# Two early expert tiles, weight splits on GpSimd and reordered gate steps in a fused attention, mixture-of-experts and dense kernel

## The chip, the cores and the metric

The kernel runs on 1 core of one Trainium2 chip. The metric is the device time of one execution in microseconds. The kernel before was run three times: 1479.68, 1479.9 and 1480.39 us, so its median is 1479.9 us.

The engines are named by their jobs: TensorE (PE in the profile) multiplies matrices and transposes, and writes to PSUM; PEld is its weight load. VectorE is DVE, ScalarE is ACT, GpSimd is POOL; SyncE (SP) only issues transfers here. A small q behind an engine's name is its instruction sequencer.

## The reference

Three stages run one after the other, all in fp32.

```python
# attention between 512 tokens and 32 states, per batch (8) and head (8), width 64
a = softmax(scale * x @ state.T);  xread = a @ state
a2 = softmax(scale * state @ x.T); sread = a2 @ x
x = concat([xread, sread], axis=2)          # -> 4352 rows of 512: 8 batches of 544

# mixture of experts: 8 experts, 512 -> 1024 -> 512, one expert per row
logits = (x / |x|) @ (emb / |emb|).T / tau
e = argmax(logits);  gate = softmax(logits)[e]
x = gate * (relu(x @ w1[e]) @ w2[e])

# dense: 512 -> 2048 -> 512
r = relu(x @ w_in)
out = (s * r * r + b) @ w_out
```

With the inputs of the reference the experts get 851, 381, 299, 441, 934, 323, 655 and 468 rows, and in tiles of 128 rows 7, 3, 3, 4, 8, 3, 6 and 4, together 38. Of the 851 rows of expert 0, 714 lie in the first six batches.

## The kernel before

**Precision by splits.** TensorE multiplies in a narrower format, so each fp32 factor is split into a hi and a lo part. ScalarE makes `hi` by a copy that rounds (`x_hi`, `win_hi`, `split_hi`, `hidden_hi`), VectorE makes `lo = raw - hi` (`x_lo`, `win_lo`, `split_lo`, `hidden_lo`), and each product is hi by hi, hi by lo and lo by hi.

**Attention.** A loop over 8 batches is pipelined over the engines. In iteration i, TensorE does the scores of batch i (L1119), the ranks of batch i-2 (`ranks`, L1221), the state read of batch i-1, `state_emb(i)`, which waits for `pos_ready` of batch i-2, the transposes of the scores (L1144), the transposes of x of batch i+1 (L1102), and the token read of batch i-1 (L1190). ScalarE copies the x transposes out, does one exp over `e1`, 128x1024 (L587), then the copy of the state row (`row_t_evac`), the copies `a2_n` and the rows of batch i-1 (`rows_evac`, L559). VectorE does `place(i-2)`, `token_rows(i-1)`, the softmax steps, `state_logits(i-1)` and `choose(i-1)`. SyncE stores the rows of each batch to `x_tok` in HBM.

**Routing.** Each batch has a stage in which `choose` finds the expert of each row, `ranks` counts with two small matmuls how many rows of this expert came before, and `place` (L803 to L809) turns this into positions `pos5`. GpSimd then scatters the row numbers to `slot_tab` in HBM by five indirect DMAs (L478), one word per row. `pos5` is one buffer, so `place(bb)` waits until the slots of all batches before bb are written:

```python
if bb >= 1:
    dve.wait_ge(slots_written, 16 * (TPB + 1) * bb)
nc.vector.tensor_scalar(pos5[:], rank5[:], float(E * CAP), None, ALU.add).then_inc(pos_ready, 1)
```

After the last batch VectorE works out a table of tiles (`tile_tab`: the expert of each tile, whether it changes after it, its slot and its first row; L905 to L935). SyncE reads `slot_tab` back into `slot_sb` (L396), TensorE transposes it (L1265), VectorE copies it to `idx_all` (L939).

**Expert stage.** 38 tiles of 128 rows. `gather(g)` on GpSimd copies one column of indices and gathers 128 rows into `xg` (L492); it waits until the transposes (`xg_tr`), the sum of squares (`gate_sq`) and the logits (`gate_lg`) of the tile before have read `xg`. On TensorE `tile(g)` is `turn_hidden(g)`, `turn_x(g + 2)` (L1276), `up(g + 1)` (L1290), `down(g)` (L1316). On VectorE, it is `x_lo(g+2)`, `next_w1(g+1)`, `gate_final(g+2)`, `gate_logits(g+3)`, `hidden_lo(g+1)`, `gate_scale(g+3)`, `next_w2(g)`. `gate_scale` is a chain of 15 small steps on one column, each waiting for the one before (L993 to L999, the rsqrt steps at L748 to L753). `gate_soft(g)` on ScalarE waits for it. At a change of expert `next_w1` and `next_w2` split the next expert's weights, four hi and four lo parts of 128x1024 each (lo at L961 and L970), and `win_hi` and `win_lo` (L952) split one eighth of the dense weights `w_in`. SyncE loads the next expert's weights into one buffer, `w_raw`, as its halves come free.

The first expert's weights are split after attention: `split_hi` on ScalarE (L546, L550), `split_lo` on VectorE (L840, L844).

**Dense stage.** Tiles of up to 512 rows, `HEAD` = 2 blocks of 128 first. GpSimd adds up the 16 blocks of `w_out` for the bias (`b_row`, L512), VectorE makes `y_lo` (L1046) and `wo_lo` (L1041), TensorE does `dense_up` (L1357) and `dense_down` (L1376). GpSimd scatters the output rows to HBM (L524), and the program ends when the last of these has landed.

## Time and profile before

| | |
|---|---|
| median of three runs | 1479.9 us |
| the profiled execution, its own time | 1480.5 us |
| its span, first to last instruction | 1478.8 us |
| mean granted TensorE clock | 0.965 of full |
| TensorE matmul busy | 1365.8 us, 92% |
| VectorE busy | 651.3 us, 44% |
| ScalarE busy | 509.1 us, 34% |
| GpSimd busy | 149.0 us, 10% |

The rows below are taken from one profiled execution on the core. Times are in microseconds from the start of the span. In a row of the timeline the first two numbers are start and length of an instruction, or of several equal ones (x4), then come engine, line, operation and tiles, and in brackets how long the engine was idle before and what ended that. In the chain a row is a piece of the path that ended last. Busy shares of TensorE's matmuls include their pipelined ends.

### The profile page before, as it was taken

How to read it: one execution, taken by the hardware profiler on the slowest of the kernel's cores; microseconds unless marked ns; L12 is line 12 of the kernel's file. 1: busy time of each engine (PE TensorE's matmuls, PEld its weight loads, DVE VectorE, ACT ScalarE, POOL GpSimd, SP SyncE). 2: the span in 40 equal slices, each digit the busy share in tenths (PEclk: the TensorE clock that was granted, in tenths of full speed). 3: DMA queues.
4: the chain of work that ended last, by engine and by line, in shares of the span. 5: the costliest groups of instructions: out<-in, count | busy, mean ns of one | idle time of the engine just before them, and what ended most of it. 6: DMA issues, size and time to landing. Idle time of an engine off the chain costs nothing.

```text
span 1478.8 us, 22719 instructions
## 1 busy us (share of the span) xinstructions
PE 1365.8 (92%) x6878; PEld 1118.7 (76%) x6879; DVE 651.3 (44%) x1646; ACT 509.1 (34%) x977; POOL 149.0 (10%) x196
## 2 busy tenths in 40 slices
PE   5887459999999999997999999999999999999995
PEld 4655338877787877876888888888888888888884
DVE  4776653566664466465632422423223232322322
ACT  3544413455453355353422222222222222222221
POOL 1222310000000000004000100101001010100101
PEclk9988669999999999999999999999999999999998
DMA  9745333144433144214010010101001010010000
GB/s 218 147 112 79 65 106 120 51 150 172 172 115 101 44 161 146 80 52 153 24 44 0 24 34 0 57 0 57 0 0 57 0 57 0 21 36 0 29 1 28
DMA packets 75154, 100.19 MB, mean 68 GB/s; under 512 B 43977, under 2 KB 44521, under 8 KB 74097
## 3 DMA queue, kind: packets, MB, share of 16 engines
q1 hardware_dynamic: 62448, 69.72, 16.7%
q0 software_dynamic: 7200, 20.08, 4.1%
q10 hardware_dynamic: 5472, 9.96, 1.8%
q8 instruction: 19, 0.31, 0.1%
q14 instruction: 15, 0.11, 0.0%
HBM read 71.24 MB, written 28.66 MB: 68 GB/s over the span
## 4 chain that ended last, share of the span: by engine, by line
PE 74%; DVE 7%; DMA 5%; issue 5%; ACT 3%; DVEq 2%; ACTq 1%; POOL 1%; SPq 0%; another core or an unknown queue 0%; POOLq 0%
PE bank_a L1357 25%; PE bank_n L1376 13%; PE bank_t L1376 12%; PE bank_a L1290 9%; PE bank_n L1316 8%; DMA xg<-x_tok,g_idx 3%; PE bank_t L1301 1%; DMA slot_tab<-ids,pos 1%; DMA x_tok<-st_rows 1%; DVEq L339 1%; PE bank_a L1102 1%; PE bank_n L1276 1%; DVEq L336 1%; PE bank_t L1119 1%; DVE w_lo L970 1%
## 5 line engine op out<-in xcount | busy, mean ns | idle before, releaser
L1054 DVE TENSOR_TENSOR sq<-rel 128x512 f32<-128x512 f32 (+1 forms) x144 | 95.5, 663 | 484.8 <-ACT rel L714 484.8
L714 ACT ACTIVATE rel<-bank_a 128x512 f32<-128x512 f32 (+1 forms) x144 | 82.8, 575 | 549.6 <-PE bank_a L1357 549.6
L1357 PE MATMUL bank_a<-y_hi,w_in_hi 128*128 128x512 f32 (+1 forms) x576 | 218.6, 379 | 7.1 <-DVE y_lo L1046 7.0
L1357 PE MATMUL bank_a<-y_hi,w_in_lo 128*128 128x512 f32 (+1 forms) x576 | 217.9, 378 | 0.0
L1357 PE MATMUL bank_a<-y_lo,w_in_hi 128*128 128x512 f32 (+1 forms) x576 | 217.8, 378 | 0.0
L1357 PEld LDWEIGHTS bank_a<-y_hi,w_in_hi 128*128 128x128 f32 x576 | 109.0, 189 | 28.7 <-DVE y_lo L1046 7.5
L1357 PEld LDWEIGHTS bank_a<-y_lo,w_in_hi 128*128 128x128 f32 x576 | 109.0, 189 | 20.7 <-issue 0.2
L1357 PEld LDWEIGHTS bank_a<-y_hi,w_in_lo 128*128 128x128 f32 x576 | 108.9, 189 | 19.9
L1316 PE MATMUL bank_n<-w_hi,hid_hi 128*128 128x512 f32 x304 | 118.4, 389 | 1.9 <-DVE hid_lo L977 1.9
L1316 PE MATMUL bank_n<-w_hi,hid_lo 128*128 128x512 f32 x304 | 118.3, 389 | 0.0
L1376 PE MATMUL bank_n<-wo_hi,g_hi 128*128 128x512 f32 x288 | 112.6, 391 | 0.2 <-DVE g_lo L1057 0.2
L1376 PE MATMUL bank_n<-wo_lo,g_hi 128*128 128x512 f32 x288 | 112.2, 390 | 0.0
L1376 PE MATMUL bank_n<-wo_hi,g_lo 128*128 128x512 f32 x288 | 112.1, 389 | 0.0
L524 POOL DMA_INDIRECT out_rows<-w_raw,out_id x34 | 36.5, 1075 | 690.2 <-DVE w_raw L1066 685.0
L1290 PE MATMUL bank_a<-w_hi,xg_hi 128*128 128x512 f32 x304 | 100.1, 411 | 1.6 <-DVE xg_lo L948 1.4
L1376 PE MATMUL bank_t<-wo_hi,g_hi 128*128 128x512 f32 x256 | 100.8, 394 | 0.0
L1376 PE MATMUL bank_t<-wo_hi,g_lo 128*128 128x512 f32 x256 | 99.7, 389 | 0.0
L1376 PE MATMUL bank_t<-wo_lo,g_hi 128*128 128x512 f32 x256 | 99.6, 389 | 0.0
L1057 DVE TENSOR_TENSOR g_lo<-sq,g_hi 128x512 fp32r<-128x512 f32 (+1 forms) x144 | 95.5, 663 | 6.7
L1290 PE MATMUL bank_a<-w_hi,xg_lo 128*128 128x512 f32 x304 | 95.9, 397 | 0.0
L1316 PE MATMUL bank_n<-w_lo,hid_hi 128*128 128x512 f32 x304 | 81.7, 400 | 8.8 <-DVE w_lo L970 8.4
L718 ACT ACTIVATE g_hi<-rel 128x512 fp32r<-128x512 f32 (+1 forms) x144 | 87.7, 609 | 4.6
(202 smaller groups left out, 2065.7 us busy)
## 6 DMA issues: line engine op xcount, KB each, us to landing
w_raw<-in_moe_w SPq DMA_DIRECT2D x16, 2048.0 KB, 9.3
moe_tok<-yg ACTq DMA_DIRECT2D x38, 256.0 KB, 2.0
x_tok<-x_rows SPq DMA_DIRECT2D x8, 1088.0 KB
x_m<-in_x SPq DMA_DIRECT2D x8, 1024.0 KB
y_rows<-moe_tok SPq DMA_DIRECT2D x8, 1024.0 KB
win_raw<-in_moe_w_in SPq DMA_DIRECT2D x8, 512.0 KB, 8.9
w_raw<-in_moe_w_out SPq DMA_DIRECT2D x1, 4096.0 KB
slot_tab<-ids,pos POOLq DMA_INDIRECT x40
```

Of the source, the lines that this page charges most:

```text
L336: return eng.value_load(tile_tab[0:1, ds(g, 1)], min_val=0, max_val=E - 1)
L339: return eng.value_load(tile_tab[0:1, ds(NSLOT + g, 1)], min_val=0, max_val=1)
L524: nc.gpsimd.indirect_dma_start(out=out[:, :], out_offset=bass.IndirectOffsetOnAxis(ap=out_id[:, r:r + 1], axis=0), in_=o_sb[:, k, :], in_o ...
L714: nc.scalar.activation(rel[:, k, 0:cols], ps_g[k][:, 0:cols], ACT.Relu).then_inc(rel_ready, 1)
L718: nc.scalar.activation(g_hi[:, k, 0:cols], rel[:, k, 0:cols], ACT.Square).then_inc(g_hi_done, 1)
L970: nc.vector.tensor_tensor(w2_lo[:, c], w_raw[:, WCOLS + k * SLOT:WCOLS + (k + 1) * SLOT], w2_hi[:, c], ALU.subtract).then_inc(w2_ready, 1)
L1054: nc.vector.tensor_tensor(sq[:, 0:cols], rel[:, k, 0:cols], rel[:, k, 0:cols], ALU.mult).then_inc(sq_ready, 1)
L1057: nc.vector.tensor_tensor(g_lo[:, k, 0:cols], sq[:, 0:cols], g_hi[:, k, 0:cols], ALU.subtract).then_inc(g_ready, 1)
L1290: last = nc.tensor.matmul(ps_h[j][:], a[:, xc], w[:, c * F + j * BANK:c * F + (j + 1) * BANK], start=(c == 0 and a is xg_hi and w is w1_hi ...
L1316: last = nc.tensor.matmul(ps_y, a[:, kc], w[:, k * D:(k + 1) * D], start=(k == 0 and a is hid_hi and w is w2_hi), stop=(k == FC - 1 and w ...
L1357: last = nc.tensor.matmul(ps_g[n % 2][:, 0:cols], w[:, wc], a[:, c, 0:cols], start=(c == 0 and w is w_in_hi and a is y_hi), stop=(c == DC ...
L1376: last = nc.tensor.matmul(ps_o[TROWS - rows + r], a[:, n % 2, rc], w[:, wc], start=(n == 0 and a is g_hi and w is wh), stop=(n == FC2 - 1 ...
```

## The change

- `EARLY` = 2 tiles are filled from the rows of the first six batches (`SOON` = 6). After the slots of batches 0 to 5 are written, SyncE reads the first 256 slots of expert 0 into `idx_soon`; GpSimd gathers tiles 0 and 1 from them, between `write_slots(6)` and `write_slots(7)`. TensorE runs `up(0)`, `up(1)`, `down(0)` and `down(1)` around the last ranks, the slot transposes and the transposes of tile 2, which stand between the hi and the lo part of one of these each. Should expert 0 have fewer than 256 rows in those batches, `room` holds the lacking number: later rows are moved behind it, and the table and the copies of the ids take it into account.
- `split_hi(i)` moves into iteration i of attention on ScalarE. `split_lo` moves from VectorE to GpSimd, in front of `write_slots(k - 2)`.
- VectorE does `gate_logits(0)` and `x_lo(0)` ahead of `choose(B - 1)`, `gate_scale(0)` ahead of `place(B - 1)`. In a tile `gate_scale(g + 2)` stands directly behind `x_lo(g + 2)`, and `gate_final` at the end.
- `win_hi` and `win_lo` move from `next_w1` to `next_w2`, and SyncE loads w2 ahead of the piece of `w_in`.
- The first rows of the dense stage are loaded ahead of `w_out`.
- In the rsqrt step `y*y*n2` is formed as `y*n2*y`.

```diff
 # SyncE
+                if bb == SOON:
+                    sp.wait_ge(slots_written, 16 * (TPB + 1) * SOON)
+                        sp.dma_start(idx_soon[:], slot_tab[0:EARLY * P, :].rearrange("(t p) o -> p (t o)", p=P)).then_inc(soon_loaded, 16)
...
-            sp.wait_ge(gathered, 16)
+            sp.wait_ge(gathered, 16 * (EARLY + 1))
+            sp.wait_ge(st_stored, 16 * B)
             load_win(0)
             for e in range(1, E):
                 sp.wait_ge(w1_ready, WS * e)
                 sp.dma_start(w_raw[:, 0:WCOLS], w1[e].rearrange("(c p) n -> p c n", p=P)).then_inc(w1_loaded, 16)
+                sp.wait_ge(w2_ready, WS * e)
+                sp.dma_start(w_raw[:, WCOLS:2 * WCOLS], w2[e].rearrange("(c p) n -> p c n", p=P)).then_inc(w2_loaded, 16)
                 sp.wait_ge(win_ready, e)
                 load_win(e)
-                sp.wait_ge(w2_ready, WS * e)
-                sp.dma_start(w_raw[:, WCOLS:2 * WCOLS], w2[e].rearrange("(c p) n -> p c n", p=P)).then_inc(w2_loaded, 16)
 # GpSimd
-            for bb in range(B):
+            def split_lo(k):
+                if k < WS:
+                    pool.wait_ge(w1_hi_done, k + 1)
+                    c = slice(k * SLOT, (k + 1) * SLOT)
+                    nc.gpsimd.tensor_tensor(w1_lo[:, c], w_raw[:, c], w1_hi[:, c], ALU.subtract).then_inc(w1_ready, 1)
+                else:
...
+            def write_slots(bb):
                 pool.wait_ge(pos_ready, bb + 1)
                 for t in range(TPB + 1):
...
+            for k in range(2 * WS):
+                split_lo(k)
+                if k >= 2:
+                    write_slots(k - 2)
+            write_slots(B - 2)
+            pool.wait_ge(soon_loaded, 16)
+            pool.wait_ge(rows_stored, 16 * SOON)
+            pool.wait_ge(st_stored, 16 * SOON)
+            gather(0)
+            gather(1)
+            write_slots(B - 1)
             pool.wait_ge(rows_stored, 16 * B)
             pool.wait_ge(st_stored, 16 * B)
+            pool.wait_ge(tab_ready, 1)
             pool.wait_ge(idx_ready, 1)
-            gather(0)
-            pool.wait_ge(tab_ready, 1)
-            gather(1)
             gather(2)
 # ScalarE, attention loop
                 nc.scalar.activation(e1[:], e1[:], ACT.Exp, scale=-1.0).then_inc(e1_done, 1)
+                split_hi(i)
                 if i >= 1:
                     row_t_evac(i - 1)
...
-            for k in range(2 * WS):
-                split_hi(k)
 # ScalarE, first tiles
+            x_hi(0)
             gate_square(0)
-            x_hi(0)
             gate_soft(0)
-            act.wait_ge(tab_ready, 1)
             gate_square(1)
             hidden(0)
             x_hi(1)
-            next_w1(0)
+            hidden_hi(0)
+            hidden(1)
+            act.wait_ge(st_stored, 16 * B)
+            result(0)
+            act.wait_ge(tab_ready, 1)
+            store(0)
+            hidden_hi(1)
+            next_w1(1)
+            x_hi(2)
 # VectorE, rsqrt step, place, end of attention
-                    link(nc.vector.scalar_tensor_tensor(t, y, y, n2, ALU.mult, ALU.mult))
+                    link(nc.vector.scalar_tensor_tensor(t, y, n2, y, ALU.mult, ALU.mult))
...
+                if bb == SOON:
+                    route_step(nc.vector.tensor_scalar(room[:, 1:2], bank_l[:, L_SUM:L_SUM + 1], float(EARLY * P), None, ALU.min))
...
+                if bb >= SOON:
+                    route_step(nc.vector.scalar_tensor_tensor(rank5[:], hot5[:, :, 0], room[:, 0:1], rank5[:], ALU.mult, ALU.add))
...
             place(B - 2)
             token_rows(B - 1)
             state_logits(B - 1)
+            dve.sem_inc(hid_t_ready, HB)
+            gate_logits(0)
+            x_lo(0)
             choose(B - 1)
+            gate_scale(0)
             place(B - 1)
+            gate_logits(1)
+            x_lo(1)
+            hidden_lo(0)
+            gate_final(0)
...
             nc.vector.tensor_copy(tile_tab[:], tab_o[:]).then_inc(tab_ready, 1)
-            for k in range(WS):
-                split_lo(k)
             dve.wait_ge(slot_tr, 1)
             nc.vector.tensor_copy(idx_all[:], bank_r[:, E:E + 3 * TQ]).then_inc(idx_ready, 1)
-            for k in range(WS, 2 * WS):
-                split_lo(k)
+            gate_scale(1)
+            hidden_lo(1)
 # VectorE, a tile
             def tile(g):
                 x_lo(g + 2)
+                gate_scale(g + 2)
                 next_w1(g + 1)
-                gate_final(g + 2)
                 gate_logits(g + 3)
                 hidden_lo(g + 1)
-                gate_scale(g + 3)
                 next_w2(g)
+                gate_final(g + 2)
 # TensorE
             turn_x(0)
-            up(0)
+            up(0, last_ranks)
+            turn_hidden(0)
             turn_x(1)
+            up(1)
+            down(0, turn_slots)
+            turn_hidden(1)
+            down(1, lambda: turn_x(2))
             pe.wait_ge(tab_ready, 1)
+            up(2)
+            turn_x(3)
             last_g = last_tile(pe)
-            tile(0)
-            with pe.Fori(1, last_g) as g:
+            with pe.Fori(2, last_g) as g:
                 tile(g)
```

The second argument of `up` and `down` is called between their hi and their lo part. Tile 0 uses other PSUM banks (`ps_xt0`, `ps_y0`). Five table steps are added behind `o_row`, and the `moe_id` copies become ten instead of eight.

## Rows read from the trace of the kernel before

**Rows 1.** The page's 40 slices of the span, TensorE: busy tenths
```profile
PE   5887459999999999997999999999999999999995
```

**Rows 2.** Windows: us, busy us (count) of each engine, PEclk, DMA
```profile
176.00:202.00 26.00, 2.10 (x8) 1.41 (x9) 16.12 (x32) 2.63 (x5) 8.27 (x9) 0.50 0.17 48
```

**Rows 3.** The chain that ended last, 157 to 203 us: start, length, what
```profile
160.93 0.18 DVE pos L809
...
166.48 8.64 DMA slot_tab<-ids,pos
...
175.22 0.18 DVE pos L809
...
180.95 8.79 DMA slot_tab<-ids,pos
...
195.01 4.19 DMA xg<-x_tok,g_idx
...
201.76 1.65 PE bank_a L1290 x3
```

**Rows 4.** Timeline of ScalarE: the exp of e1 in batches 2, 5, 6, 7
```profile
55.40 1.06 ACT L587 ACTIVATE e<-e 128x1024 f32<-128x1024 f32 x1
...
111.86 1.05 ACT L587 ACTIVATE e<-e 128x1024 f32<-128x1024 f32 x1
...
130.93 1.06 ACT L587 ACTIVATE e<-e 128x1024 f32<-128x1024 f32 x1 [0.63 <-issue]
...
150.60 1.06 ACT L587 ACTIVATE e<-e 128x1024 f32<-128x1024 f32 x1 [4.70 <-DVE e L869]
```

**Rows 5.** Timeline of GpSimd and VectorE: slot scatters and pos
```profile
57.20 0.87 POOL L478 DMA_INDIRECT slot_tab<-ids,pos  x1 [0.30 <-issue]
...
68.04 0.17 DVE L809 TENSOR_SCALAR pos<-rank 128x5 int32<-128x5 f32 x1 [0.30 <-DMA slot_tab<-ids,pos]
...
125.64 0.17 DVE L809 TENSOR_SCALAR pos<-rank 128x5 int32<-128x5 f32 x1
...
151.07 0.86 POOL L478 DMA_INDIRECT slot_tab<-ids,pos  x1 [0.30 <-issue]
```

**Rows 6.** GpSimd's adds for b_row: ns min/median/max, first and last start
```profile
L512 POOL TENSOR_TENSOR b_row<-b_row,w_raw x14: 1262/1274/1607, 686.0 to 703.6; 128x512 f32<-128x512 f32 x14
```

**Rows 7.** Timeline of GpSimd: the last scatter of output rows
```profile
1468.17 0.97 POOL L524 DMA_INDIRECT out_rows<-w_raw,out_id  x1 [0.30 <-issue]
```

**Rows 8.** Timeline of TensorE: lo part of up(0), transposes of gathered tiles
```profile
208.37 1.98 PE L1290 MATMUL bank_a<-w_lo,xg_hi 128*128 128x512 f32 x8
...
228.80 0.60 PE L1276 MATMUL bank_n<-ident,xg 128*128 128x128 f32 x4
...
241.01 0.60 PE L1276 MATMUL bank_n<-ident,xg 128*128 128x128 f32 x4
...
302.18 0.60 PE L1276 MATMUL bank_n<-ident,xg 128*128 128x128 f32 x4
...
316.92 0.60 PE L1276 MATMUL bank_n<-ident,xg 128*128 128x128 f32 x4
```

**Rows 9.** Timeline of VectorE: gate_scale and w2 splits at a change
```profile
306.00 0.15 DVE L993 TENSOR_REDUCE gc<-lg 128x1 f32<-128x8 f32 x1
...
309.13 0.17 DVE L999 RECIPROCAL gc<-gc 128x1 f32<-128x1 f32 x1
...
310.75 4.63 DVE L970 TENSOR_TENSOR w_lo<-w_raw,w_hi 128x1024 fp32r<-128x1024 f32 x4 [1.46 <-ACT w_hi L631]
```

**Rows 10.** Timeline of VectorE and TensorE ahead of the dense stage
```profile
694.17 1.33 DVE L751 SCALAR_TENSOR_TENSOR gc<-gc 128x1 f32<-128x1 f32 x1
...
701.91 0.69 DVE L1046 TENSOR_TENSOR y_lo<-bank_r,y_hi 128x512 fp32r<-128x512 f32 x1 [1.79 <-issue]
...
690.50 0.49 PE L1316 MATMUL bank_n<-w_hi,hid_hi 128*128 128x512 f32 x1 [1.90 <-DVE hid_lo L977]
...
703.25 0.58 PE L1357 MATMUL bank_a<-y_hi,w_in_hi 128*128 128x256 f32 x1 [7.03 <-DVE y_lo L1046]
```

More of the change, by code:

```diff
@@ L379, in _ @@
                 sp.dma_start(x_tok[bb * ROWS + S:bb * ROWS + ROWS, :], st_rows[:]).then_inc(st_stored, 16)
+                if bb == SOON:
+                    sp.wait_ge(slots_written, 16 * (TPB + 1) * SOON)
+                    with nc.allow_non_contiguous_dma(reason="one word per row"):
+                        sp.dma_start(idx_soon[:], slot_tab[0:EARLY * P, :].rearrange("(t p) o -> p (t o)", p=P)).then_inc(soon_loaded, 16)
             w_in_s = w_in.rearrange("(c p) n -> p c n", p=P)
@@ L503, in _ @@
             gather(3)
-            with pool.Fori(1, last) as g:
+            gather(4)
+            with pool.Fori(2, last) as g:
                 gather(g + 3)
@@ L668, in _ @@
             x_hi(1)
-            next_w1(0)
+            hidden_hi(0)
[7 more added lines that the diff above has]
+            x_hi(2)
             gate_soft(1)
             gate_square(2)
-            hidden_hi(0)
+            result(1)
+            store(1)
+            gate_soft(2)
+            gate_square(3)
+            hidden(2)
+            x_hi(3)
+            next_w1(2)
+            gate_soft(3)
+            hidden_hi(2)
+            gate_square(4)
             win_hi(0)
+            next_w2(1)
             last = last_tile(act)
@@ L685, in tile @@
                 next_w2(g)
-            tile(0)
-            with act.Fori(1, last) as g:
+            with act.Fori(2, last) as g:
                 tile(g)
@@ L1013, in _ @@
             gate_scale(1)
-            x_lo(1)
-            next_w1(0)
+            hidden_lo(1)
+            next_w1(1)
+            gate_logits(2)
+            x_lo(2)
             gate_final(1)
-            gate_logits(2)
             gate_scale(2)
-            hidden_lo(0)
+            gate_logits(3)
+            gate_final(2)
+            x_lo(3)
+            gate_scale(3)
+            next_w1(2)
+            hidden_lo(2)
+            gate_logits(4)
             win_lo(0)
+            next_w2(1)
@@ L1021, in _ @@
+            gate_final(3)
             last = last_tile(dve)
@@ L1024, in tile @@
                 x_lo(g + 2)
+                gate_scale(g + 2)
                 next_w1(g + 1)
-                gate_final(g + 2)
                 gate_logits(g + 3)
                 hidden_lo(g + 1)
-                gate_scale(g + 3)
                 next_w2(g)
-            tile(0)
-            with dve.Fori(1, last) as g:
+                gate_final(g + 2)
+            with dve.Fori(2, last) as g:
                 tile(g)
@@ L1259, in _, with last_ranks, turn_slots @@
             row_logits(B - 1)
-            ranks(B - 1)
-            nc.tensor.matmul(bank_r[:, 0:E], ones_b[:], pre5[:, TPB + 1, :], start=True, stop=True).then_inc(tot_mm, 1)
-            pe.wait_ge(slot_loaded, 16)
-            pe.wait_ge(tab_link, 1)
-            for k in range(3):
-                last = nc.tensor.transpose(bank_r[:, E + k * TQ:E + (k + 1) * TQ], slot_sb[:, k, :], ident[0:TQ, 0:TQ])
-            last.then_inc(slot_tr, 1)
+            def last_ranks():
+                ranks(B - 1)
+                nc.tensor.matmul(bank_r[:, 0:E], ones_b[:], pre5[:, TPB + 1, :], start=True, stop=True).then_inc(tot_mm, 1)
+            def turn_slots():
+                pe.wait_ge(slot_loaded, 16)
+                pe.wait_ge(tab_link, 1)
+                for k in range(3):
+                    last = nc.tensor.transpose(bank_r[:, E + k * TQ:E + (k + 1) * TQ], slot_sb[:, k, :], ident[0:TQ, 0:TQ])
+                last.then_inc(slot_tr, 1)
             def turn_x(g):
@@ L1302, in turn_hidden, with down @@
                     last.then_inc(hid_tr, 1)
-            def down(g):
-                e = 0 if starts(g) else expert_of(pe, g)
-                if not starts(g):
+            def down(g, between=None):
+                e = 0 if isinstance(g, int) and g < EARLY else expert_of(pe, g)
+                if starts(g):
+                    pe.wait_ge(pos_ready, B)
+                elif not (isinstance(g, int) and g < EARLY):
                     pe.wait_ge(yg_ready, g)
+                dst = ps_y0 if starts(g) else ps_y
                 for w, done, factors in ((w2_hi, w2_hi_done, (hid_hi, hid_lo)), (w2_lo, w2_ready, (hid_hi,))):
+                    if between and w is w2_lo:
+                        between()
                     for k in range(FC):
```

204 lines of the change are left out of this document (116 added, 88 removed).

## The prediction

> **What bounds the kernel now.** I read the page of the profile first: TensorE is busy nine tenths or more from slice 7 to the end, with a hole in slices 4 and 5 and a dent in slice 18 [rows 1]. The windows size the hole: from 176 to 202 us TensorE works 2.1 of 26 us, at half clock [rows 2]. The chain says what fills it: position numbers, slot scatter, its landing, read-back, index, gather, first expert tile [rows 3]. Outside that, the expert stage has a steady period of 228.80 to 241.01 = 12.21 us, longer at the seven changes of expert [rows 8], and before the dense stage TensorE waits 7.03 us [rows 10]. The attention stage is not bound by TensorE: it is a loop over several engines, in which the exp of `e1` on ScalarE comes once a batch (call its start X, counted X2 for i = 2) [rows 4].
>
> **Splits in attention.** Eight hi halves move into attention behind that exp. They have the exp's shape, 128x1024, so 1.06 us each [rows 4]. The eight lo halves move from VectorE, where they lay under the slot wait (so removing them gives nothing), to GpSimd. Nearest row: 128x512 on GpSimd takes 1.27 us [rows 6], so 2.55 us each; bounds 1.3 (no growth with size) and 3.2 (twice its slowest, 1.607).
>
> What matters is who queues behind them. In GpSimd's order `write_slots(k-2)` now stands behind `split_lo(k)`, which waits for `split_hi(k)`, which runs after exp of batch k. Before, the fifth scatter of a batch was issued 5.55 us after `pos` (160.93 to 166.48 [rows 3]), thus about at X. Now `pos` has long been there, and GpSimd gets to it at X + 1.06 (exp) + 1.0 (split hi) + 2.55 = X + 4.6; the fifth goes out some 5.5 later, at X + 10.1. It then has to land, and `place(bb)` still waits for all slots of the batches before bb ahead of writing `pos5`. Landing, from the start of the fifth issue: 8.64 and 8.79 us in the chain [rows 3]; 10.8 in batch 0 (from 57.20 to the wait of `pos` that ended at 68.0, under other transfers); at most 9.9 for batch 5 (151.07, and `pos` at 160.93 did not wait) [rows 3, 5]. Another scatter, of the output, also has 10.6 us from its issue to the end of the span [rows 7]. I take L = 9.2, bounds 8.64 and 10.8.
>
> In batch i+1, `place(i-1)` thus ends at X(i) + 10.1 + L, where before it ended 13.8 us after X (111.86 to 125.64). TensorE's `state_emb` waits for `pos`, and the score transposes and x transposes behind it lead to the next exp: 125.64 to 130.93 = 5.2 us [rows 4, 5]. So the period becomes 15.3 + L = 24.5 us, against 19.1 and 19.7 before (111.86, 130.93, 150.60 [rows 4]). From X2 = 55.40 + 1 = 56.4: four periods to X6 = 154.2, one shorter by 1.05 (the last has no x transposes) to X7 = 177.6, before 150.60. After the loop, `place(6)` waits for slots of batch 5: 177.6 + 10.1 + 9.2 = 196.9, where before it was 160.93. This is **+36** (L = 8.64: +32.6; 10.8: +45.6). Without this wait the hi splits alone would have given some +7.
>
> By the Trainium skill, page "DMA: Bandwidth & Descriptors", section "Anatomy of one DMA", a GpSimd DMA costs about 2 us plus its bytes; the period would stay below 20 us and this term would be 7. The trace's 8.64 and 8.79 disagree with it, and I go by them.
>
> **Early tiles.** Expert 0 has 714 rows in six batches (counted from the reference's inputs), over 256, so `room` is 0 and there are still 38 tiles. What they gain is TensorE work under the last slot wait. From `pos` of batch 6 (p): five scatter issues 6.5, index copy and its hand-over 1.3, then from the gather's issue to the first matmul 6.75 (195.01 to 201.76 [rows 3], of it 4.19 the landing) give the start T of `up(0)` at p + 14.6; p + 20 if the gather queues behind the slot scatter. VectorE now waits for that gather before `choose(7)`, which waited for no gather before: all the last routing comes behind it. `last_ranks` comes behind the hi part of `up(0)`, 6.6 us at half clock (201.76 to 208.37 [rows 3, 8]), so the last `pos` is at T + 8.0. From there to the next gathered tile (now tile 2) it took 24.0 (175.22 to 195.01 + 4.19 [rows 3]): T + 32.0. Under it TensorE does `up(0)`, `up(1)`, `down(0)`. Then a second wait: VectorE copies the indices at T + 26.4 and only then does `gate_scale(1)`, 3.3 us (306.00 to 309.13 + 0.17 [rows 9]), and `hidden_lo(1)`; `down(1)` starts at T + 31, runs 5.5 (under half a period of 12.21) plus the transposes between its halves, `up(2)` starts at T + 37. It runs 5.5, and gathers 3 and 4, each released only by the transposes before it, put the transposes ahead of `up(3)` at T + 47.6 = p + 62.2. Before, that point was 241.01 - 160.93 = 80.1 after p [rows 3, 8]. Gain **-17.9**. The five extra table steps and two more `moe_id` copies lie under these waits; uncovered they would cost 1.2 and a few us.
>
> So the stage ends 36 - 18 = **+18** later (bounds +14.7 and, with L = 10.8 and the queued gather, +33).
>
> **Changes of expert.** Before, the transposes at 302.18 and 316.92 lie 14.74 apart, 2.5 over the period; TensorE waits for `w_lo` of w2, whose four splits start at 310.75 behind `gate_scale` (3.3 us) [rows 8, 9]. With `gate_scale(g+2)` moved ahead of them they start about 1.9 earlier (gather and `gate_soft` come 1.4 later, which eats the rest of 3.3). `win_lo` now stands behind them and before the next `x_lo`: 1.2 us (a quarter of the 4.63 of the four splits), which takes back 0.8. Seven times 1.1 = **-8** (bounds 0 and -17.7, the whole excess). In a plain tile ScalarE's chain is longer by the waited `gate_soft`; `hidden_hi` comes 2 us later and still 0.9 before `down` needs it, so nothing. If that cover is short, 31 tiles pay it.
>
> **Dense start.** TensorE waits until 703.25 because the last `gate_scale` is stretched: its steps with two inputs take 1.3 us (694.17) rather than 0.2 while GpSimd adds up `b_row`, and `y_lo` comes at 701.91 [rows 10]. The same steps now come before `hidden_lo(37)`, just as the adds start: the stretch delays `down(37)` instead, from 690.5 [rows 10] to some 697, and the dense stage starts 1 to 2 us earlier. **-1.5** (bounds -7.03, stretch gone; +2). The earlier row loads were done in time before: nothing.
>
> The Trainium skill, page "GPSIMD Engine Reference", section "Key points", says that GpSimd contends with VectorE instructions of two SBUF inputs. The trace agrees (1.30 us against 0.22); by that rule the new operand order of the rsqrt step, still two inputs, changes nothing here.
>
> **Sum.** 1480.5 (the profiled run, span 1478.8 plus 1.7) + 18 - 8 - 1.5 = 1489.0; the median of the runs is 0.6 below the profiled one, so 1488.
>
> **Rivals.**
> 1. *The gather queues behind the slot scatter and landings are 10.8*: 1480.5 + 33 - 8 - 1.5 = 1504. For: 10.8 was seen under load. Against: scatters are issued 1.27 us apart and yet land together.
> 2. *Faster: the scatters land in time.* If L is 5 or less, `place` no longer waits in the loop (period 15.3 + L against the 20 of the loop with splits). Then attention gives +7, the last slot landing is 5 us shorter, and the stage ends 16 earlier: 1480.5 - 16 - 8 - 1.5 = 1455. What the Trainium skill's page says of about 2 us would be this case. Against: four rows between 8.64 and 10.8. It turns into a gain from L = 6 or so downwards.
> 3. *Faster: forecast path, but the changes and the dense start give all they can*: +14.7 - 17.7 - 7 = 1470.5.
> 4. *No change*: +14.7, 2.0 saved per change, 1.6 at the dense start: 1480.
>
> **Numbers.** Forecast 0.50, rival 1 0.15, rival 2 0.10, rival 3 0.12, rival 4 0.08; 0.05 for a stall that I don't see, slower. About 0.2%, 3 us, is what a measurement can tell: slower 0.70, same 0.08, faster 0.22. The range 1470 to 1509 leaves out rival 2 and some 0.05 above; the forecast alone spans 1483 to 1499.
>
> **What would show it.** Right: exps of `e1` some 24 us apart from batch 2 on; VectorE's `pos` waiting for `slot_tab` in batches 3 to 7; the last exp near 178; `up(0)` near 211 with a wait for slots inside `down(0)`; transposes at a change 13.6 apart. Wrong: periods of 20 us (the landing is hidden, rival 2); `pos` waiting over 11 us; a plain tile above 12.3 us, from the later `hidden_hi`; the stretched steps gone from VectorE.

## The result and the profile after

The kernel after takes 1558.7 us (median of 4, 1557.0 to 1561.0), the kernel before 1479.8 on the same chip: ratio 1.0534, 95% interval 1.0516 to 1.0553. It is slower, as forecast, but by 79 us where 8 were forecast, and outside the range. The profiled span is 1556.8 us against 1478.8, 78.0 more.

TensorE's row of the page's 40 slices (tenths busy in slices of 38.9 us) shows where:

```profile
PE   3754663799999999999799999999999999999995
```

Slices 0 to 6 are now thin, not only 4 and 5 [rows 1]; from slice 8 on the page looks as before. The windows give batches 2 to 6 in one row (length, busy us and count of PE, PEld, DVE, ACT and POOL, granted clock, DMA share, GB/s):

```profile
74.00:220.00 146.00, 82.10 (x664) 61.51 (x664) 73.80 (x175) 50.27 (x112) 36.09 (x30) 0.74 0.48 65
```

TensorE is busy 56% of the time, and no engine more. Where no engine is near full, the engines wait for one another in a circle. Two timelines and the chain close it: the exp of `e1` on ScalarE (compare [rows 4]), `pos` on VectorE, and one batch of the chain.

```profile
37.70 1.05 ACT L635 ACTIVATE e<-e 128x1024 f32<-128x1024 f32 x1
...
73.50 1.05 ACT L635 ACTIVATE e<-e 128x1024 f32<-128x1024 f32 x1
104.34 1.05 ACT L635 ACTIVATE e<-e 128x1024 f32<-128x1024 f32 x1
136.13 1.06 ACT L635 ACTIVATE e<-e 128x1024 f32<-128x1024 f32 x1
163.59 1.05 ACT L635 ACTIVATE e<-e 128x1024 f32<-128x1024 f32 x1
...
219.46 1.06 ACT L635 ACTIVATE e<-e 128x1024 f32<-128x1024 f32 x1 [13.68 <-DVE e L927]
```

```profile
97.48 0.17 DVE L877 TENSOR_SCALAR pos<-rank 128x5 int32<-128x5 f32 x1 [11.81 <-DMA slot_tab<-ids,pos]
129.72 0.17 DVE L877 TENSOR_SCALAR pos<-rank 128x5 int32<-128x5 f32 x1 [13.00 <-DMA slot_tab<-ids,pos]
157.19 0.17 DVE L877 TENSOR_SCALAR pos<-rank 128x5 int32<-128x5 f32 x1 [7.41 <-DMA slot_tab<-ids,pos]
...
242.15 0.17 DVE L877 TENSOR_SCALAR pos<-rank 128x5 int32<-128x5 f32 x1 [10.41 <-DMA slot_tab<-ids,pos]
267.57 0.17 DVE L877 TENSOR_SCALAR pos<-rank 128x5 int32<-128x5 f32 x1
```

The chain that ended last (start, length, what) runs once round the circle:

```profile
136.13 0.47 ACT e L635
...
137.08 1.07 ACT w_hi L598
...
138.22 2.34 POOL w_lo L505
...
140.72 1.00 POOL slot_tab L512
...
145.94 11.16 DMA slot_tab<-ids,pos
...
157.19 0.18 DVE pos L877
...
157.51 0.60 PE bank_l L1201 x8
158.11 1.90 PE bank_n L1213 x8
160.01 2.52 PE bank_a L1171 x12
...
163.59 0.48 ACT e L635
```

Read it as exp, hi split, lo split, five scatters, landing, `pos`, score and x transposes, exp. The periods are 30.8, 31.8, 27.5, 28.3 and 27.6 us.

Three points of the span split the 78.0 us. `pos` of batch 6 comes at 242.15 instead of 160.93 [rows 3]: **+81.2**. The transposes ahead of up(3) come 69.3 us after it (row below) instead of 80.1 [rows 3, 8]: **-10.7**. From there to the last gathered tile it is 439.7 us instead of 434.3, **+5.4**, and from there to the first product of `dense_down` 34.9 instead of 32.6, **+2.3**. The rest is equal.

```profile
296.64 0.60 PE L1352 MATMUL bank_n<-ident,xg 128*128 128x128 f32 x4
306.41 0.66 PE L1352 MATMUL bank_n<-ident,xg 128*128 128x128 f32 x4 [1.02 <-DMA xg<-x_tok,g_idx]
311.49 0.66 PE L1352 MATMUL bank_n<-ident,xg 128*128 128x128 f32 x4 [2.69 <-DMA xg<-x_tok,g_idx]
```

### The profile page after: what moved, and what is told of

The parts are those of the page before. It is cut to its first block, busy times and chain, and to the rows that moved or that the text cites. A ratio compares the mean times of both kernels' runs of the same rounds, so it can differ in the third digit from the quotient of the medians.

```text
span 1556.8 us, 22584 instructions
## 1 busy us (share of the span) xinstructions
PE 1385.7 (89%) x6879; PEld 1133.9 (73%) x6880; DVE 660.3 (42%) x1633; ACT 508.1 (33%) x977; POOL 169.7 (11%) x208
## 4 chain that ended last, share of the span: by engine, by line
PE 64%; DMA 9%; issue 7%; DVE 6%; ACT 5%; POOL 3%; ACTq 3%; SPq 1%; DVEq 1%; POOLq 0%
PE bank_a L1448 24%; PE bank_n L1467 13%; PE bank_t L1467 11%; PE bank_n L1401 6%; PE bank_a L1370 5%; DMA slot_tab<-ids,pos 5%; DMA xg<-x_tok,g_idx 4%; POOL slot_tab L512 2%; PE bank_a L1171 1%; DVE gc L813 1%; ACTq L345 1%; PE bank_t L1381 1%; PE bank_n L1213 1%; DVE gc L815 1%; ACTq L348 1%
## 5 line engine op out<-in xcount | busy, mean ns | idle before, releaser
L1401 PEld LDWEIGHTS bank_n<-w_hi,hid_hi 128*128 128x128 f32 x296 | 57.2, 193 | 36.4 <-issue 22.1
## 6 DMA issues: line engine op xcount, KB each, us to landing
x_tok<-x_rows SPq DMA_DIRECT2D x8, 1088.0 KB, 10.1
```

Of the source, the lines that this page charges most:

```text
L1401: last = nc.tensor.matmul(dst, a[:, kc], w[:, k * D:(k + 1) * D], start=(k == 0 and a is hid_hi and w is w2_hi), stop=(k == FC - 1 and w i ...
```

## The experiments

Of a1 to a4, b1 and e3 there is one execution each, and only terms of several us are read from it: three of the kernels below have the same attention code and reach `pos` of batch 6 at 164.8, 167.5 and 172.0 us. Chips differ too: the kernel before took 1479.8 us on the chip of the result, 1476.5 on that of a1 to a4, so a difference of 2 or 3 us in their spans is not read. Times are told beside that of the kernel before on the same chip; the kernel after is 78.9 above it.

**A late start (a1).** VectorE's first reduction stands in the timeline with this wait, which the prediction had not seen:

```profile
32.43 1.28 DVE L914 TENSOR_REDUCE nb<-s_t 128x1 f32<-128x512 f32 x2 [12.92 <-POOL late L495]
```

VectorE waits for three new memsets on GpSimd, and these stand behind GpSimd's wait for the cleared slot table. The edit puts the memsets first:

```
-            pool.wait_ge(tab_cleared, 16)
             nc.gpsimd.memset(first_e[:], 0.0).then_inc(tab_zero, 1)
             ...
+            pool.wait_ge(tab_cleared, 16)
```

> The changed kernel, with the four small memsets for first_e and late ahead of GpSimd's wait for the cleared slot table instead of behind it. Theory (a wait that the forecast missed: VectorE's first attention step waits for these memsets, and they wait for the transfer that clears slot_tab): the first exp of e1 returns from 37.70 to about 26, and the whole is 11 to 12 us shorter, 1546. Rival (the start is late because of the loads, and the memsets lie under them): the first exp stays near 37 and the time near 1558.

Measured: 1543.4 us beside 1476.5, so 66.9 above the kernel before instead of 78.9; the span is 15.1 shorter than after. The first exp is at 25.01 (37.70 after, 25.85 before), and the theory holds. The late start costs more than itself: the next two periods are 14.56 and 16.30 us here (14.56 and 14.99 before) and were 17.63 and 18.17 after, with a granted clock of 0.94 from 25 to 56 us here and 0.78 from 37 to 74 after. X2 is at 55.87, 17.6 sooner than after (e3 below, also without the late start, has it at 56.24).

**Who stands first on GpSimd (a2).**

```
             for k in range(2 * WS):
-                split_lo(k)
                 if k >= 2:
                     write_slots(k - 2)
+                split_lo(k)
```

> The changed kernel, with write_slots(k-2) ahead of split_lo(k) in GpSimd's order. Theory (the slot scatter standing behind the split is what stretches attention): pos waits for no slots any more in batches 3 to 7, the exps of e1 come 18 to 21 us apart instead of 27 to 32, pos of batch 6 comes near 187 instead of 242.15, and the time is 50 to 58 us shorter, about 1503. Rival (the splits themselves, the hi half on ScalarE and the contention of GpSimd with VectorE, stretch it): the periods stay above 25 us and the time above 1540.

Measured: 1499.0 us beside 1476.5, 22.5 above it instead of 78.9, so 56 us less (59.5 in the span) from swapping two lines. `pos` of batch 6 is at 182.04, the periods are 19 to 21 us. In its timeline of VectorE `pos` waits for no slot any more:

```profile
103.67 0.17 DVE L877 TENSOR_SCALAR pos<-rank 128x5 int32<-128x5 f32 x1
123.64 0.17 DVE L877 TENSOR_SCALAR pos<-rank 128x5 int32<-128x5 f32 x1
144.63 0.17 DVE L877 TENSOR_SCALAR pos<-rank 128x5 int32<-128x5 f32 x1
```

**The same order on the kernel before (e3).** It gets the splits in attention and nothing else of the change: the `split_hi(i)` behind the exp, and on GpSimd

```
+            for k in range(2 * WS):
+                split_lo(k)
+                if k >= 2:
+                    write_slots(k - 2)
```

> The kernel before with one part of the change alone: the splits of expert 0 in the attention loop, the low half on GpSimd ahead of the slots of batch k-2. There is no late start here and there are no early tiles. My theory, that this order alone makes the cycle exp, split, slots, landing, positions, exp: periods of 27 to 31 us, the positions of batch 6 some 55 us later than 160.9, and the time 1525 to 1535 us. The rival, that the early tiles' traffic or the added waits lengthen the landings: periods as forecast (24.5 us) and 1510 to 1516 us.

Measured: 1542.8 us beside 1477.1. `pos` of batch 6 is at 225.91, 65.0 us later than [rows 3]; the periods are 28 to 32 us. Two landings in its chain:

```profile
157.50 12.94 DMA slot_tab<-ids,pos
...
187.00 12.74 DMA slot_tab<-ids,pos
```

So the order alone makes the circle and its long landings. My number for `pos` was 10 us too small and the time lies 8 us above my range; the mechanism and place are right, and the rival (traffic of the early tiles) is out: there are none here, and the landings are 10.9 to 15.6 us, 13.2 on average.

**Why the landing is long (a4).** After, the scatters of a batch (140.72 to 145.94) go out together with SyncE's store of 1088 KB of token rows (issued at 141.96, median 10.1 us to landing; 5.9 in a2). The edit holds that store, and with it what SyncE has queued behind it (the state row and the next load of x), until the slots of the batches before are written:

```
+                if bb >= 1:
+                    sp.wait_ge(slots_written, 16 * (TPB + 1) * bb)
                 sp.dma_start(x_dst(bb), x_rows[:]).then_inc(rows_stored, 16)
```

> The changed kernel, with SyncE's store of the rows of a batch waiting until the slots issued before it have landed, so that scatter and store are no longer in flight together. Theory (the scatters land in 11 to 15 us instead of 8.6 to 8.8 because they now meet the row store): from the fifth issue to the end of pos's wait falls to about 9 us. Rival (they land late for a reason of their own): it stays at 12 or more. The time itself gets longer under both, by 5 to 50 us, since the store is now on the path of each batch.

Measured: 1548.7 us beside 1476.5, 72.2 above it instead of 78.9, span 9.8 *shorter*, against my forecast of longer. From the fifth issue to the end of the wait of `pos`:

| batch | 1 | 2 | 3 | 4 | 5 | 6 | mean |
|---|---|---|---|---|---|---|---|
| after | 14.1 | 15.6 | 11.3 | 12.4 | 12.4 | 12.9 | 13.1 |
| a4 | 8.8 | 7.3 | 6.0 | 12.9 | 10.5 | 8.0 | 8.9 |

```profile
118.79 0.17 DVE L879 TENSOR_SCALAR pos<-rank 128x5 int32<-128x5 f32 x1 [2.85 <-DMA slot_tab<-ids,pos]
143.90 0.17 DVE L879 TENSOR_SCALAR pos<-rank 128x5 int32<-128x5 f32 x1 [2.16 <-DMA slot_tab<-ids,pos]
175.78 0.17 DVE L879 TENSOR_SCALAR pos<-rank 128x5 int32<-128x5 f32 x1 [8.43 <-DMA slot_tab<-ids,pos]
```

(The table's a4 for batch 6 is 222.56 to 230.57.) With SyncE's transfers out of the way the landings are some 4 us shorter on average. The counts of DMA packets in windows show what the transfers do, and what they don't. In a4 the last packet of a scatter has moved 2 to 3 us after the fifth issue; after, with the store under way, 128 of the 160 packets of batch 4 move together between 176 and 177 us, up to 3.6 us after the issue at 173.38, and in the other batches the last ones move 4 to 8 us after it. Behind that comes a stretch of 4 to 11 us in which no packet of the scatter moves, in both kernels, before the wait of `pos` ends. It is what makes batch 4 of a4 long (windows 163 to 165 and 165 to 175.7 us; the wait ends at 175.78):

```profile
q0 software_dynamic: 64, 0.00, 2.0%
...
DMA packets 1, 0.01 MB, mean 1 GB/s; under 512 B 0, under 2 KB 0, under 8 KB 0
```

(The one packet is an instruction fetch. In the kernel before there is no packet at all from 184 to 189.7 us, the end of the landing of 8.79 [rows 3].) So SyncE's transfers explain some 4 of the 13.1 us. The longer part passes with none of the scatter's packets left to move, and why it takes 4 us once and 11 another time is open.

Of the 4.2 us gained per landing about 1.9 per batch reach `pos` of batch 6 (11.6 us sooner in all), for the path goes over the held queue now: the store of the state row stands behind the held one, and the next exp comes 8.3 to 9.3 us after `pos` instead of 5.4 to 6.9. From a4's chain:

```profile
137.86 5.94 DMA slot_tab<-ids,pos
...
144.23 4.80 DMA x_tok<-st_rows
```

**The order of the gate (a3).** VectorE's `gate_scale` goes back a tile ahead, `win_*` stays in `next_w2`:

```
             def tile(g):
                 x_lo(g + 2)
-                gate_scale(g + 2)
                 next_w1(g + 1)
+                gate_final(g + 2)
                 gate_logits(g + 3)
                 hidden_lo(g + 1)
+                gate_scale(g + 3)
                 next_w2(g)
-                gate_final(g + 2)
```

> The changed kernel, with VectorE's order in a tile as before (gate_final, gate_logits, hidden_lo, then gate_scale of the next tile but one), win_hi and win_lo still in next_w2. Theory (the new place of gate_scale loads the tiles around a change of expert and the last tile): excess over 12.25 us a tile falls from 23 to 18 or less, TensorE's 9.53 us wait in down of the last tile goes, total 5 to 8 us shorter, 1551. Rival (win_lo and the load order cause it): no more than 2 us.

Measured: 1556.1 us beside 1476.5, 79.6 above it; against my 5 to 8 us there is no gain that the times can tell. In the trace the excess over 12.25 us a tile falls from 23.2 to 22.2 us only, not to 18. At a change of expert, three intervals between transposes are 12.98, 12.88 and 13.64 us after, and 14.57, 12.86 and 12.25 in a3. Both are about 3 above the plain 36.75, where before it was 2.7. With `gate_scale` back, TensorE waits for `w_lo` as in the kernel before; with it ahead of the splits, ScalarE waits for the last step of `gate_scale`, with `gate_square`, `result` and `hidden_hi` queued behind, and TensorE then waits for `hid_lo` (0.74 us at 395.72). From the kernel after:

```profile
374.53 0.30 ACT L695 ACTIVATE pr<-sh,gc 128x8 f32<-128x8 f32 x1 [3.97 <-DVE gc L1001]
...
391.39 0.30 ACT L695 ACTIVATE pr<-sh,gc 128x8 f32<-128x8 f32 x1 [5.15 <-DVE gc L1001]
```

What a3 does mend is the dense start. After, the stretched gate steps stand ahead of `hidden_lo(37)` (VectorE, then TensorE):

```profile
763.74 1.30 DVE L813 SCALAR_TENSOR_TENSOR gc<-gc 128x1 f32<-128x1 f32 x1
765.26 1.12 DVE L815 TENSOR_TENSOR gc<-gc 128x1 f32<-128x1 f32 x1
```

```profile
773.99 0.79 PE L1401 MATMUL bank_n<-w_hi,hid_hi 128*128 128x512 f32 x1 [9.53 <-DVE hid_lo L979]
```

In a3 this wait is 1.90 us as before, and from the last gathered tile to the end it takes 803.3 us, before 803.5, after 805.6.

**The dense rows alone (c3).** The kernel before with `load_y(0, HEAD)` and `load_ids(0, HEAD)` ahead of the load of `w_out`.

> The kernel before, with only the loads of the first dense rows and their ids ahead of the load of the last weights. The prediction gave this part 1.5 us and no more than 7. Now I expect nothing: within 1 us of the kernel before, since TensorE waited 7.03 us at the first dense product for VectorE's y_lo, and after the change still 9.5 us for VectorE's hid_lo at the same place. The rival: 1.5 us or more faster.

Measured: ratio 1.0001 (0.9989 to 1.0013). Nothing, as the prediction's last sentence on the dense start had it.

**The terms together (b1, b2).** b1 is a1 and a2 in one kernel, b2 adds a3.

> The two largest terms taken away together: the small memsets ahead of the wait for the cleared table, and GpSimd writing the slots of batch k-2 before it splits piece k. If they are separate terms of the sum, they add: 1499.0 - 11.9 to 15 = about 1485 to 1487 us. The rival, that the late start was partly hidden behind the slot waits or behind the time of x: over 1492 us.

> The same with VectorE's gate_scale back a tile ahead, as before the change, in the loop over tiles. Two costs are then out of b1: ScalarE's waits for VectorE's reciprocal at a change of expert (some 0.2 us per change and one for up(3)), and gate_scale in the way of hid_lo at the start of the dense part (2.4 us). Expected 3 us below b1, about 1482 us, so level with the kernel before (1476.5 to 1480 us). The rival, that gate_scale costs only while the routing is late: the same as b1.

Measured: b1 1487.2 us beside 1482.5, 4.7 above it. a1 and a2 alone took off 12.0 and 56.4 of the 78.9, which would leave 10.5: together they are worth at least their sum. b2 1481.0 beside 1482.5, ratio 0.9992 (0.9976 to 1.0007). With three orders put right the whole change is worth nothing that can be measured.

**Where the lo split runs (b3).** From GpSimd back to VectorE, into its idle time between `r2` and the exp of `e1`:

```
                 nc.vector.reciprocal(r2[:], s2[:]).then_inc(sum2_steps, 1)
+                if i >= 1:
+                    split_lo(i - 1)
```

> b2 with the low halves split on VectorE, in its idle time before ScalarE's exp, instead of on GpSimd. My theory for what is left of the longer attention stage (some 1.3 us per batch): GpSimd's 2.34 us split stretches VectorE's small sum step from 0.18 to 2.1 us, and what follows waits for it. Then this step is back at 0.18 us, the batches are some 1 us shorter each, and the time is 6 to 9 us below b2. The rival, that ScalarE's 1.05 us high half ahead of its row copies is what lengthens a batch: no more than 2 us below b2, or above it, since VectorE has 1.23 us more in each batch.

Measured: ratio 0.9994 (0.9979 to 1.0008), the same as b2. The stretch is real and costs nothing that shows; in b2 and in b3 the small step is

```profile
97.07 2.12 DVE L936 TENSOR_SCALAR s<-s 128x32 f32<-128x32 f32 x1
```

```profile
97.76 0.18 DVE L936 TENSOR_SCALAR s<-s 128x32 f32<-128x32 f32 x1
```

and yet both have `pos` of batches 2 and 3 18.8 us apart (89.29 and 108.10; 90.03 and 108.83). My theory fell: the stretched step stood in the timeline, but the batch waits for something else, and for what was not followed up.

**The moved splits alone, slots first (e2).** e3 with the two lines swapped.

> The same part with the slots ahead of the split. It prices the moved splits alone, and so what the early tiles are worth in the kernel with three parts put right, which is level with the kernel before: there the path from the positions of batch 6 to up(3)'s transposes was 69.0 us against 80.1. If the early tiles give those 11 us by themselves, and the splits in attention cost 4 us and give nothing behind it, this kernel is 2 to 5 us slower than the kernel before. The rival, that part of the 11 us comes from the splits being out of the way behind the routing: level with the kernel before or faster.

Measured: ratio 1.0003 (0.9980 to 1.0027). `pos` of batch 6 is at 162.92, and up(3) 76.9 us behind it. So of the 11 us that b2 gains against 80.1 on that path, 3.2 come with the splits out of the way (2.5 in e3), 7.9 with the early tiles. b2 then loses 4.7 us of it again in the expert stage (439.4 us against 434.7), 2.1 of them in its first tile, 14.3 us long. That tile is long after too. The windows show a granted clock of 0.87 ahead of it, with TensorE busy 75%, 0.89 in it, and full speed (2.4 GHz) only from the next tile on; before, the same tile ran at 1.00. Below 1 the clock was for a part of the stretch at its lower level, 1.2 GHz:

```profile
258.00:311.00 53.00, 39.87 (x166) 30.58 (x166) 27.01 (x121) 12.48 (x30) 9.45 (x13) 0.87 0.38 135
```

```profile
311.00:326.00 15.00, 14.18 (x61) 11.61 (x62) 7.59 (x31) 4.94 (x13) 1.79 (x3) 0.89 0.18 54
326.00:338.00 12.00, 12.00 (x60) 10.03 (x59) 5.20 (x22) 4.21 (x11) 1.15 (x2) 1.00 0.17 52
```

**The gathers and the last routing (b4, c1, c2, e1, f1, g1).** After, the chain behind `pos` of batch 6 begins with this row, more than twice the 4.19 of [rows 3]:

```profile
249.03 9.28 DMA xg<-x_tok,g_idx
```

All six kernels start from b2. b4 puts `choose(7)` ahead of `gate_logits(0)` on VectorE and the last ranks ahead of tile 0 on TensorE.

> b2 with the choice of the last batch put ahead of the work of tile 0 on VectorE, and its ranks ahead of tile 0 on TensorE. My theory for the part of the early tiles' gain that did not come: VectorE and TensorE wait for gather(0), 9.3 us after its issue, with the last routing queued behind it. Then the last positions come some 8 to 11 us sooner, the last slots are issued right behind gather(1), about 5 us sooner, and so is up(3): 4 to 6 us below b2. The rival, that the two early tiles themselves fill that time: the same as b2.

Measured: 1478.9 us beside 1482.5, ratio 0.9968 (0.9948 to 0.9988), 2 us below b2 and not the 4 to 6 expected. The choice is done at 184.5, but the last `pos` comes only at 194.87, since `place(7)` still stood behind the gate of tile 0. Half the step was moved. c1 moves `place(7)` too, and the last slots ahead of the second gather:

```
             gather(0)
-            gather(1)
             write_slots(B - 1)
+            gather(1)
```

> The kernel with the choice first, but the last batch's routing is now finished ahead of tile 0 on every engine: VectorE places it before the logits of tile 0, and GpSimd writes its slots before it issues gather(1). There the choice was done at 184.5 us, and the positions still came at 194.87, behind the gate of tile 0. I expect the last positions some 8 us sooner, the slots in place some 7 us sooner, gather(1) some 1.5 us later and landing behind the slots; up(3)'s transposes 5 to 8 us sooner than 67 us after the positions of batch 6, so about 60, and the time 1471 to 1474 us where the kernel before has 1480. The rival, that gather(1), now behind the slots in its queue, holds up tile 1 by as much: no gain.

Measured: 1485.9 us beside 1482.8, ratio 1.0020 (1.0003 to 1.0037): slower, just clear of the noise, where 1471 to 1474 was expected; the rival had it. The last `pos` is 14.0 us behind that of batch 6 instead of 22.9, and it is all given back, because now gather(1) too is behind five scatters:

```profile
175.96 8.94 DMA xg<-x_tok,g_idx
...
190.58 9.48 DMA xg<-x_tok,g_idx
```

c2 puts gather(0) ahead of the slots of batch 6 and leaves gather(1) behind those of batch 7.

> c1 with gather(0) ahead of the slots of batch 6 on GpSimd, so that it has the queue for itself. If its 9.3 us to landing come from the five slot writes ahead of it, it lands some 4 us after its issue, about 10 us sooner, and tile 0 starts right behind the last ranks: 3 to 4 us below c1. If the landing stays near 9 us, it is the traffic of the row store, and c2 is 1 us below c1 or equal to it.

Measured: ratio 1.0025 (1.0009 to 1.0042), no better than c1 where 3 to 4 us were expected. gather(0) no longer holds anybody up; gather(1), issued at 190.80, takes 9.83 us and does. It is not the row store that holds it: no packet of SyncE's queue moves from 187 to 199 us. e1 puts both ahead: gather(0), slots of 6, gather(1), slots of 7.

> Gathers and slots in an order that keeps each gather clear of slots just issued: gather(0), slots of batch 6, gather(1), slots of batch 7, with the last batch placed ahead of tile 0 on VectorE and TensorE. In the kernels that were level or slower, a gather issued behind five slot writes landed 9.3 to 9.8 us later, one on a quiet queue 3.4 to 4.7 us later. So I expect gather(1) to land within 5 us, tile 1 to start some 10 us sooner than in c1, the last slots to be in place by 32 us after the positions of batch 6, and up(3)'s transposes about 60 us after them: 1470 to 1474 us, faster than the kernel before by 0.4% or more. The rival, that something behind the slots holds up tile 2 (the index table, the store's wait): up(3) at 66 to 70 us and level with the kernel before.

Measured: 1472.6 us beside 1477.1, ratio 0.9979 (0.9957 to 1.0001): half of the 0.4% expected, and not clear of no change. gather(1), issued at 178.27 with the slots behind it, has landed at 181.75, 3.5 us later. But `pos` of the last batch waits for the slots of batch 6, which went out behind a gather, with `x_lo(0)` queued behind it (VectorE's timeline):

```profile
177.05 0.17 DVE L877 TENSOR_SCALAR pos<-rank 128x5 int32<-128x5 f32 x1 [4.60 <-DMA slot_tab<-ids,pos]
```

And gather(3) meets the loads of the next weights (4.5 MB, issued from 206.25 on):

```profile
211.84 8.09 DMA xg<-x_tok,g_idx
...
221.63 3.39 DMA xg<-x_tok,g_idx
```

f1 holds these loads until gather(3) has landed:

```
-            sp.wait_ge(gathered, 16 * (EARLY + 1))
+            sp.wait_ge(gathered, 16 * (EARLY + 2))
```

> The kernel with the gathers kept clear of the slots, and SyncE's loads of w_in and of expert 1's weights (4.5 MB, 206 to 221 us) held until gather(3) has landed instead of gather(2). There gather(3), issued at 211.84 in the middle of them, took 8.09 us to land where the next one took 3.4, and up(3) waits for it. Expected: gather(3) in 3.4 to 4 us, up(3)'s transposes 4 us sooner (61 us after the positions of batch 6 instead of 65), and the weights still in time for the first change of expert: ratio to the kernel before 0.995, about 1470 us against 1477. The rival, that gather(4) meets the loads instead and tile 4 waits as long: no gain.

Measured: 1473.7 us beside 1474.9, ratio 0.9996 (0.9977 to 1.0015). The rival holds: gather(3), issued at 213.53, has landed at 217.45, gather(4) meets the loads and takes 6.84. g1 is e1 with tile 0 ahead of the last placing on VectorE:

```
             choose(B - 1)
-            place(B - 1)
             gate_logits(0)
             x_lo(0)
+            place(B - 1)
             gate_scale(0)
```

> The kernel with the gathers kept clear of the slots, and VectorE's logits and lo half of tile 0 moved ahead of the last batch's placing. In that kernel VectorE waited 4.60 us in pos for the slots of batch 6 (172.5 to 177.05), with x_lo(0) queued behind it, and TensorE 5.50 us for x_lo(0) at the start of up(0). Expected: up(0) some 4 us sooner, gather(1) too, the last slots 1 us sooner, and up(3)'s transposes 3 to 4 us sooner (61 to 62 us after the positions of batch 6): ratio to the kernel before about 0.995. The rival, that up(3) hangs on the landing of the last slots and not on the tiles ahead of it: 1 us, and a ratio of 0.998 as without it.

Measured: 1470.1 us beside 1476.5, ratio 0.9955 (0.9929 to 0.9982): faster than the kernels before and after. From `pos` of batch 6 to the transposes ahead of up(3), in the profiled runs:

| after | b2 | b4 | c1 | c2 | e1 | f1 | g1 |
|---|---|---|---|---|---|---|---|
| 69.3 | 69.0 | 67.0 | 71.9 | 76.1 | 65.1 | 67.8 | 61.7 |

g1 reaches the p + 62.2 of the prediction (p is `pos` of batch 6), by another order: there `choose(7)` does not wait for a gather.

## Why the prediction was wrong

**The circle was right, its size was not.** `pos` of batch 6 was forecast at 196.9 and came at 242.2, 45.3 us later. By the terms of that sum:
- X2 at 73.50 instead of 56.4: 17.1. This is the late start, a wait that the prediction did not see at all and so put at nothing; I had read what the new memsets compute, not what GpSimd was waiting for ahead of them. 11.85 are the first exp, the rest are the longer batches 1 and 2 behind it. With the memsets moved, X2 is at 55.87 (a1), and the 1 us allowed for the hi splits was right.
- The landing L. The step says "I take L = 9.2, bounds 8.64 and 10.8"; measured 13.1 on average, in six batches 23.5 us. All four rows it rested on [rows 3, 5, 7] are of scatters in another place of the loop. In the landing of 8.64 the row store was issued 3.3 us behind the fifth scatter (169.78); moved to 4.6 us behind the exp, the scatters have it issued among them, 4.0 us ahead of the fifth (141.96 and 145.94), and their packets move later. With SyncE's transfers held the mean is 8.9 (a4), close to the 9.2. The upper bound was a landing "under other transfers" already, and still too low by 2. Most of each landing, though, passes without a packet, and its length is not explained (a4).
- From `pos` to the next exp 6.2 us on average instead of 5.2 (last 4.15): 6.2 in all. In this stretch TensorE had a granted clock of 0.74 and was busy 56%; from 75 to 151 us of the kernel before it had 0.82 and was busy 80%. That the clock is the cause of the 6.2 was not tested.
- The fifth scatter at X + 9.8, forecast X + 10.1: -1.7 in six batches. The added pieces (1.0 us hi, 2.34 lo against 2.55) were priced right.

17.1 + 23.5 + 6.2 - 1.7 = 45.1. The sum itself has a slip of 0.2 (four periods of 24.5 from 56.4 end at 154.4, not 154.2), which changes nothing. The prediction's own sign of being wrong, "`pos` waiting over 11 us", came in batches 1 and 2.

**Early tiles: -10.7 instead of -17.9.** The step that failed is "p + 14.6; p + 20 if the gather queues behind the slot scatter" with 14.6 chosen: gather(0) takes 9.28, 5.1 more, and `up(0)` starts at p + 18.7. `choose(7)`, which the prediction had put behind that gather, is late with it. From there to the transposes ahead of `up(3)` it takes 50.6 instead of 47.6, of which gather(3) with 6.72 makes 2.5. The term counted gathers at 4.19, the price on a quiet queue. With the gathers ahead of the slots, and `choose(7)` ahead of one, a gain as large as the forecast 17.9 is there (g1: 80.1 - 61.7 = 18.4, of which some 3 come with the splits out of the way, e2).

**Changes of expert: +5.4 in the stage instead of -8.** The step that failed is "Seven times 1.1": `gate_scale` ahead of the w2 splits did start them sooner (5.4 us behind the tile's transposes at 375.65 instead of 8.6 behind those at 302.18), but the excess of a change stayed, at 2.8 to 3.6 us in six of the seven. The cost went over to ScalarE, which now waits 4 to 5 us for the reciprocal ahead of `hidden_hi`. With `gate_scale` back and `win_*` moved it is 2.9 (a3): neither order gains. The prediction had the queue right ("`gate_soft` come 1.4 later") and looked for the damage in plain tiles alone. 2.2 of the 5.4 us are the first tile, at the lower clock (0.89).

**Dense start: +2.3 instead of -1.5**, just beyond the bound of +2. That "the stretch delays `down(37)`" was right, by some 6.5 us; measured from the last gathered tile it is 7.7 (22.8 instead of 15.2), and after 9.53 us of waiting TensorE runs the first products of `down(37)` in 0.63 us each instead of 0.39. a3 gives back 2.3. The moved loads give nothing (c3), as forecast. Nor does the new operand order of the rsqrt step: it still takes 1.30 us beside GpSimd's adds.

45.1 + 7.2 + 13.4 + 3.8 = 69.5, and the profiled run is 69.5 above the sum (1558.5 against 1489.0).

**The rivals.** Landings in time (1455) is excluded by a2 and e3: the wait was there and cost 56 to 60 us. (By the prediction's own sum this rival turns into a gain from L = 7.8 downwards; at its "L = 6 or so" only the stage does, without the 9.5 of the later terms.) Rival 1 had both of its halves right, queued gather and long landing, and stopped at 10.8. Its "yet land together" holds of the wait alone: in the kernel before the packets move one scatter after another (32, 32, 20 and 12 in the four us from 165). By the Trainium skill, page "DMA: Bandwidth & Descriptors", section "Anatomy of one DMA", about 2 us would be the fixed part of such a transfer; here one-word scatters took 5.6 to 15.6 us to land (b2, after) and a gather on a quiet queue 3.3 to 4.2, so it priced neither.

## What to carry to other kernels

An instruction put into an engine's order ahead of one that others wait for costs not its own 2.3 us but the cycle that it closes: ask what the moved-in instruction waits for (here an exp of the same batch), and who waits for what now stands behind it. Put the short DMA issues that others wait for first and the filler work last; here this is a swap of two lines worth 56 to 60 us. A duration of a transfer read at one place of a loop is not its duration at another, so when an issue moves, list what is in flight at its new place before taking the old row. And a gain on the path that ends last has to be followed to the next shared queue: 9 us gained at the last positions were given back to one gather behind five scatters.

The early tiles are sound: with the orders of a1, a2, a3 and g1 put right the change is worth 0.45% (0.9955, interval 0.9929 to 0.9982).

## What was not expected of the hardware

- GpSimd's 128x1024 subtraction stretches a 128x32 step of VectorE with one SBUF input from 0.18 to 2.12 us, about to the end of the GpSimd instruction, not by a share of it (b2 against b3).
- A gather issued directly behind five one-word scatters in GpSimd's queue landed 8.9 to 9.8 us after its issue, each time (after, b4, c1 twice, c2); with the scatters behind it 3.5 (e1), alone 3.3 to 4.2.
- A gather of 128 rows beside 4.5 MB of weight loads in another queue took 6.4 to 8.1 us (after, b2, b4, c1, c2, e1, f1); after, the DMA engines' busy share was 1.00 from 299.7 to 306.3 us.
- Between the last packet of a one-word scatter and the end of the wait for it 4 to 11 us pass in which the core's DMA queues can be empty (5.7 us in the kernel before, and 10.7 us but for one instruction fetch in batch 4 of a4). A page's packet counts and a landing are two different things.
